# Channel mixing in three blocks of 512 tokens instead of four of 384

## What is computed

```python
def _moe2_ref(x, w_tok1, w_tok2, w_ch1, w_ch2):
    xt = x.transpose(0, 2, 1)
    h = np.maximum(xt @ w_tok1, 0.0) @ w_tok2
    u = x + h.transpose(0, 2, 1)                    # (2, 768, 384)
    h2 = np.maximum(u @ w_ch1, 0.0) @ w_ch2         # 384 -> 1536 -> 384, each token by itself
    return u + h2
```

## Time and profile before

| | us |
|---|---|
| median of 3 runs | 404.29 (404.11 to 404.49) |
| the profiled execution, device time | 401.82 |
| its span in the trace | 400.3 |

### The profile page before, as it was taken

One profiled execution on the slowest core, in us unless ns is written; L12 is line 12 of the kernel. 1 busy time (PEld: TensorE's weight loads), 2 busy tenths in 40 slices (PEclk: granted clock), 3 DMA queues, 4 the chain that ended last, 5 costly groups with the idle time before them and its releaser, 6 DMA issues.

```text
span 400.3 us, 6830 instructions
## 1 busy us (share of the span) xinstructions
PE 390.5 (98%) x2628; PEld 377.3 (94%) x2628; DVE 185.5 (46%) x392; ACT 115.1 (29%) x227; POOL 166.9 (42%) x185
## 2 busy tenths in 40 slices
PE   6899999999999999999999999999999999999997
PEld 5799988989899999899999999999999999999996
DVE  6798988667744453305444835351131023103301
ACT  4277644655401020763002131330131013002200
POOL 6687898576225670894999950000000000000000
PEclk9999999999999999999999999999999999999999
DMA  9999599543200211002123400000100100000001
GB/s 147 179 206 228 104 191 193 130 89 100 79 2 7 73 35 46 2 0 80 39 79 98 137 6 0 2 2 20 39 2 0 41 20 2 20 21 20 2 20 39
DMA packets 60145, 25.03 MB, mean 63 GB/s; under 512 B 51152, under 2 KB 58192, under 8 KB 60112
## 3 DMA queue, kind: packets, MB, share of 16 engines
q1 hardware_dynamic: 60112, 24.58, 28.8%
HBM read 22.22 MB, written 2.36 MB: 61 GB/s over the span
## 4 chain that ended last, share of the span: by engine, by line
PE 93%; DVE 3%; issue 1%; DMA 1%; POOL 1%; SPq 0%; ACT 0%; DVEq 0%; POOLq 0%
PE bank L1121 25%; PE bank L1122 25%; PE bank L1123 25%; PE bank L1225 4%; PE bank L1180 3%; PE bank L1135 3%; PE bank L1221 2%; PE bank L1262 2%; PE bank L1204 1%; DMA rc<-in_r 1%; PE bank L1190 1%; DVE suf L891 1%; PE bank L1280 1%; PE bank L1322 1%; DVE am L932 0%
## 5 line engine op out<-in xcount | busy, mean ns | idle before, releaser
L794 ACT ACTIVATE ha_hi<-bank 128x384 fp32r<-128x384 f32 x48 | 23.6, 492 | 113.1 <-PE bank L1123 113.1
L1039 DVE SCALAR_TENSOR_TENSOR ha_lo<-bank,ha_hi 128x384 fp32r<-128x384 f32 x48 | 26.8, 558 | 50.2 <-ACT ha_hi L794 50.2
L1121 PE MATMUL bank<-c_hi,ha_lo 128*128 128x384 f32 x144 | 48.2, 335 | 0.0
L1122 PE MATMUL bank<-c_lo,ha_hi 128*128 128x384 f32 x144 | 48.1, 334 | 0.0
L1123 PE MATMUL bank<-c_hi,ha_hi 128*128 128x384 f32 x144 | 48.1, 334 | 0.0
L1123 PE MATMUL bank<-u2T_hi,c_hi 128*128 128x384 f32 x144 | 48.1, 334 | 0.0
L1121 PE MATMUL bank<-u2T_hi,c_lo 128*128 128x384 f32 x144 | 48.1, 334 | 0.0
L1122 PE MATMUL bank<-u2T_lo,c_hi 128*128 128x384 f32 x144 | 48.1, 334 | 0.0
L1044 DVE TENSOR_TENSOR x<-bank,x 128x384 f32<-128x384 f32 x12 | 6.7, 558 | 65.3 <-PE bank L1123 65.3
L1121 PE MATMUL bank<-sg_hi,z_lo 128*128 128x384 f32 x96 | 32.5, 338 | 0.0
L1122 PE MATMUL bank<-sg_lo,z_hi 128*128 128x384 f32 x96 | 32.1, 334 | 0.0
(11 more groups left out here) (145 smaller groups left out, 888.7 us busy)
## 6 DMA issues: line engine op xcount, KB each, us to landing
raw<-in_moe_w_ch SPq DMA_DIRECT2D x12, 384.0 KB, 3.1
kc<-in_k SPq DMA_DIRECT2D x12, 192.0 KB, 4.5
rc<-in_r SPq DMA_DIRECT2D x12, 192.0 KB, 5.1
vn<-in_v SPq DMA_DIRECT2D x12, 192.0 KB, 5.2
raw<-in_moe_w_sg SPq DMA_DIRECT2D x6, 384.0 KB, 4.1
out<-x SPq DMA_DIRECT2D x12, 192.0 KB, 1.9
raw<-in_moe_w_in SPq DMA_DIRECT2D x4, 384.0 KB, 5.8
raw<-in_moe_w_tok SPq DMA_DIRECT2D x4, 384.0 KB, 3.3
```

Source lines behind the costliest of these rows:

```text
L794: sc.activation(ha[0][:, i, :], bank[:, 0:HALF], ACT.Relu).then_inc(act_out, 1)
L1039: ve.scalar_tensor_tensor(ha[1][:, i, :], bank[:, 0:HALF], 0.0, ha[0][:, i, :].bitcast(F32), ALU.max, ALU.subtract).then_inc(dve_out, 1)
L1121: te.matmul(dst, left[1], right[0], start=first, stop=False)
L1122: te.matmul(dst, left[0], right[1], start=False, stop=False)
```

## The change

- Three blocks of `WIDE` = 512 tokens (`NB` = 3) over both sequences in one row of 12 token tiles; a block has `BT` = 4 token tiles. The second block takes the last two token tiles of sequence 0 and the first two of sequence 1.
- `u2T[0]` holds two blocks (three rows of 1024 tokens, from Z to GT), `u2T[1]` the third, behind `ha`. `u2T_place` says where a `uT` job writes, `u2T_block` what a `ch1` job reads.
- `ha` is a pair of 12x512, from GT to ATT + 1536, so that it reaches over `wo`, `vf` and the start of `x1`; `u2T[1]` starts there and ends at `k1`.
- A `ch1` job has nine matmuls of 512 columns; there are 3 x 12 jobs instead of 4 x 12. The relu and the rest are taken of 128x512. The last token tile on which block b waits is 4b+3 of the 12.
- A block has four `ch2` jobs instead of three; their number (12) and form stay. The order becomes `ch1` 0, `uT` of sequence 1, `ch2` 0, `ch1` 1, `ch2` 1, `ch1` 2, `ch2` 2.

```diff
+WIDE = 512
+NB = B * S // WIDE
+BT = WIDE // PART
...
-        + [("ch1", 0, i) for i in range(12)] + [("uT", 1, i) for i in range(6)] + [("ch2", 0, i) for i in range(3)]
-        + [("ch1", 1, i) for i in range(12)] + [("ch2", 1, i) for i in range(3)]
-        + [("ch1", 2, i) for i in range(12)] + [("ch2", 2, i) for i in range(3)]
-        + [("ch1", 3, i) for i in range(12)] + [("ch2", 3, i) for i in range(3)])
+        + [("ch1", 0, i) for i in range(NCF)] + [("uT", 1, i) for i in range(6)] + [("ch2", 0, i) for i in range(BT)]
+        + [("ch1", 1, i) for i in range(NCF)] + [("ch2", 1, i) for i in range(BT)]
+        + [("ch1", 2, i) for i in range(NCF)] + [("ch2", 2, i) for i in range(BT)])
...
-    ha = pair("ha", GT, [PART, NCF, HALF])
+    ha = pair("ha", GT, [PART, NCF, WIDE])
...
-    u2T = [pair("u2T0", Z, [PART, KC, S]), pair("u2T1", ATT, [PART, KC, S])]
+    u2T = [pair("u2T0", Z, [PART, KC, 2 * WIDE]), pair("u2T1", ATT + 2 * NCF * WIDE - (ATT - GT), [PART, KC, WIDE])]
...
+        def u2T_place(g):
+
+            half, g = divmod(g, 2 * BT)
+            return u2T[half], slice(PART * g, PART * g + PART)
+
+        def u2T_block(b):
+            return u2T[b // 2], slice(WIDE * (b % 2), WIDE * (b % 2) + WIDE)
...
-            for q in range(4):
-                for i in range(3):
-                    b, tc = q // 2, 3 * (q % 2) + i
+            for q in range(NB):
+                for i in range(BT):
+                    b, tc = divmod(BT * q + i, NC)
...
-                    sc.activation(ha[0][:, i, :], bank[:, 0:HALF], ACT.Relu).then_inc(act_out, 1)
+                    sc.activation(ha[0][:, i, :], bank[:, :], ACT.Relu).then_inc(act_out, 1)
...
-                    ve.scalar_tensor_tensor(ha[1][:, i, :], bank[:, 0:HALF], 0.0, ha[0][:, i, :].bitcast(F32),
+                    ve.scalar_tensor_tensor(ha[1][:, i, :], bank[:, :], 0.0, ha[0][:, i, :].bitcast(F32),
                                             ALU.max, ALU.subtract).then_inc(dve_out, 1)
...
-                    dst = x[:, b // 2, 3 * (b % 2) + i, :]
+                    dst = x[:, (BT * b + i) // NC, (BT * b + i) % NC, :]
...
-                    wait_dve_out(pe, "uT", b // 2, 3 * (b % 2) + 2)
+                    wait_dve_out(pe, "uT", (BT * b + BT - 1) // NC, (BT * b + BT - 1) % NC)
+                    right, at_ = u2T_block(b)
                     for kc in range(KC):
-                        ins = three(bank[:, 0:HALF], cut(c1[kc], tile(i)), cut(u2T[b // 2], kc, tile(b % 2, HALF)),
-                                    kc == 0, kc == KC - 1)
+                        ins = three(bank[:, :], cut(c1[kc], tile(i)), cut(right, kc, at_), kc == 0, kc == KC - 1)
```

More of the change, by code:

```diff
@@ L766, in take_job @@
                         act.wait_ge(x_out, NCH - YR)
-                    dst = (xT if kind == "xT" else u2T)[b][0]
-                    sc.copy(dst[:, :, PART * i:PART * i + PART], bank[:, 0:C].rearrange("p (a t) -> p a t", a=KC)
-                            ).then_inc(act_out, 1)
+                    dst, at_ = (xT[b], slice(PART * i, PART * i + PART)) if kind == "xT" else u2T_place(NC * b + i)
+                    sc.copy(dst[0][:, :, at_], bank[:, 0:C].rearrange("p (a t) -> p a t", a=KC)).then_inc(act_out, 1)
                 elif kind == "v":
@@ L1002, in take_job @@
                     wait_act_out(dve, kind, b, i)
-                    at_ = slice(PART * i, PART * i + PART)
-                    dst = (xT if kind == "xT" else u2T)[b]
+                    dst, at_ = (xT[b], slice(PART * i, PART * i + PART)) if kind == "xT" else u2T_place(NC * b + i)
                     ve.tensor_tensor(dst[1][:, :, at_], bank[:, 0:C].rearrange("p (a t) -> p a t", a=KC),
```

## The result

The changed kernel takes 402.15 us in the median of 18 runs (400.82 to 404.43), against 404.19 us (402.38 to 405.88, 18 runs) for the kernel before beside it: a ratio of 0.996 with an interval of 0.9944 to 0.9975, so 1.0 to 2.3 us less. Forecast were 403.0 and 1.26 us less. The profiled execution, forecast at 400.56 us with a span of 399.0, took 400.82 with 399.3.

A forecast was written before the change was run, and what follows sets the result against it. The prediction took TensorE's own matmul pace as the bound. 1.44 us from 108 fewer matmuls less 0.18 for width switches gave 1.26 us less, 404.29 to 403.03, said as 403.0; range 402.5 to 403.5 us.

The forecast's parts named there:

- The bound: Channel mixing from 245.5 us: TensorE's own pace sets the time; TensorE waits for nothing and is busy 98% of the span.
- exactly 108 paces: `ch1` before the change: 108 matmuls in 18.72 us at 173.3 ns each, read as no gaps between jobs.
- The fixed part: Every matmul on TensorE costs 13.3 ns beside its columns, at 384 and 512 columns; 108 fewer matmuls gain 1.44 us.
- the term of the sum: `ch1` after the change: 324 matmuls at 226.7 ns, 73.44 us, against 74.88 us before.
- The switches: Width changes between `ch1` and `ch2`: three in at 0.04 us, two directly out at 0.03; loss 0.18 us.
- What was costed at nothing: `ch2` unchanged, bank emptying hidden under TensorE, `uT` and weights ready in time, new memory layout without added waits: 0 each.
- hand-over: From `ch1` to `ch2`: the last inner tile is needed 5.7 us after `ch2` starts; slack over 3.5 us, so 0.
- A: Rival: in `ch1` the per-matmul fixed cost is smaller or grows with columns; gain 0.3 us or less, 404.0; chance 8%.
- B: Rival: wide `ch1` matmuls slow while ScalarE and VectorE read whole banks; 0.2% slower needs 233.6 ns; 405.7 at 235; 3%.
- C: Rival: width changes cost nothing or run the other way; full 1.44 us gain, 402.85; counted within the forecast's 89%.
- D: Rival: the change does nothing because saved weight loads were hidden anyway; 404.3, counted with A, whose chance is 8%.
- The step that failed: Whole kernel: runs' median stands 2.47 us above the profiled execution; carried over unchanged, giving 404.29 - 1.26 = 403.03 us.

The follow-up runs named there:

- w256: The changed kernel with each `ch1` job as two halves of 256 columns, 18 matmuls instead of 9; a `ch1` stage took 25.91 us, 120.0 ns per matmul.
- w128: The changed kernel with each `ch1` job as four quarters of 128 columns, 36 matmuls instead of 9; the whole run took 474.27 us.
- again3: The changed kernel unedited, in a further comparison beside the kernel before; median 402.46 us (12 runs) against 404.27, ratio 0.9972.
- double: The changed kernel with ScalarE's relu of each `ch1` job done twice, the second waiting for the first; `ch1` 1 took 24.52 us.
- again: The changed kernel repeated unedited beside the kernel before; median 402.16 us (12 runs) against 403.34, ratio 0.9989.
- again2: The changed kernel unedited, in another comparison beside the kernel before; median 402.56 us (12 runs) against 403.59, ratio 0.9964.

## Why the prediction was right, and where it was not

- **The bound.** That TensorE's own pace is the time of the stage held: no wait of TensorE appeared, and doubling ScalarE's relu did nothing. The prediction's "exactly 108 paces" was no proof of it, because the pace of 173.3 ns had been taken from the same 18.72 us; the missing waits and the one line through three widths speak for it.
- **The fixed part**, 13.3 ns, held at 512 and was confirmed at 256 columns. Three `ch1` stages of 24.52 us less three times 0.04 are 73.44 us, the term of the sum. It does not hold at 128 columns.
- **The switches**: 0.04 and 0.03 us, as taken, in all five places; repeating them ten more times gave 0.33 us for 0.35.
- **What was costed at nothing** (`ch2`, emptying, hand-over, `uT`, weights, layout) was nothing. VectorE's part took 692 ns for 687, ScalarE's 598 for 598.
- **Rivals.** A falls with the pace of 226.7 in all three stages. B falls by the same, although ScalarE and VectorE now both read whole banks. C is off by the switches, which are real. D falls with the stage's 1.28 us. B's threshold of 233.6 ns leaves out the 0.18 us of the switches, which its 405.7 counts; with them it is 233.0.
- **The step that failed** is the last of the sum: "The median of the runs stands 2.47 us above the profiled execution; that difference lies outside the stage, and I carry it over". It does lie outside the stage, but it is no constant: in the first comparison it was 404.19 - 401.82 = 2.37 us for the kernel before and 402.15 - 400.82 = 1.33 us for the changed one. By the traces it is made of stretches at 1.2 GHz, 1.54 and 1.50 us for one each, and of where tile 1 starts (over 1.65 us). Each set of runs draws these anew: the medians of the kernel before itself went from 403.34 to 404.29. The profile I read happened to be of an execution at full clock, in which none of this is seen. A median of three runs within 0.4 us looked tighter than it was, and "the new ones will too" failed with it: the new runs go from 400.82 to 404.43. The gain was sized right (1.26 for 1.28 in the trace, 1.33 over all runs); in the medians of the first comparison it is 2.04. The absolute 403.0 is too high by the carried term; 404.29, where it started, is itself a median that more runs put at 403.6. By difference or ratio the forecast stands inside the first comparison's interval; in microseconds the range was too narrow by 0.35.

## What to carry to other kernels

When TensorE has no idle time, count its matmuls and not only their columns: each costs a fixed 13.3 ns here down to 256 columns, so a loop re-cut from 384 to 512 columns wins 108 x 13.3 ns, less a few hundredths for each change of width, and a cut to 128 loses far more than the line says. Read the pace from starts in the timeline; the recorded durations (334, 390 and 188 ns) show none of it. Before trusting a median to a microsecond, sort the runs by granted clock, and compare traces from a start behind the disturbance: from `ch1` 0 to the end they agree to 0.02 us here. Where a stretch at the lower clock follows an idle gap of TensorE, try matmuls that fit into the gap: here that was worth about as much as the change.

## Not expected of the hardware

- The surcharge at a switch shows only around 512 columns. Between 256 and 384 there is none: in `w256` `ch1` 1 is 216 x 120.0 and `ch2` 1 is 350.71 - 325.75 = 24.96 us, 144 x 173.3. At 512 columns the weight loads have idle time (4.2 us in each of the three groups of 108), at 384 none:

```profile
L1129 PEld LDWEIGHTS bank<-u2T_hi,c_lo 128*128 128x128 f32 x108 | 20.3, 188 | 4.2
L1131 PEld LDWEIGHTS bank<-u2T_hi,c_hi 128*128 128x128 f32 x108 | 20.3, 188 | 4.2
```

  That the surcharge comes from loads that go from back to back to waiting and back is only argued; no run tested it.
- The pairs of `w128` take 111.5 ns, although 128 columns at 2.4 GHz take 53. It is no floor for every pair: the 16 recorded pairs of the scores of tile 1, whose weights have 128 columns on 48 partitions, in turn from partition 0 and from 64 on, take 18.90 - 17.81 = 1.09 us in the changed kernel's trace, 68 ns each.
- Whether the clock falls after the same idle of 1.4 us differs from run to run of one kernel. The four traces with a fall near 18 us start tile 1 at 17.07 to 17.55; the three that start it at 18.67 to 18.72 (`again3`, `double`, `w128`) have none there and one near 45; `again` at 17.51 and the changed kernel at 17.81 have neither. The fall near 45 follows no idle as long as that one (0.19 us in the trace of `again2`). Why it falls there, and why filling the idle near 17 us helps against it, stays open.
